# Expert weights loaded in DMAs of 128 columns

## What is computed

```python
xn = x / (np.linalg.norm(x, axis=-1, keepdims=True) + 1e-06)
logits = xn @ en.T / tau
expert_idx = np.argmax(logits, axis=1)
for e in range(E):
    mask = expert_idx == e
    h = np.maximum(x[mask] @ w1[e], 0.0)        # w1: 8 x 512 x 1024
    out[mask] = gate_w[mask, None] * (h @ w2[e]) # w2: 8 x 1024 x 512
```

## Time and profile before

| | us |
|---|---|
| median of 3 runs | 1424.7 |
| lowest and highest | 1419.62, 1425.99 |
| profiled execution, its own time | 1430.08 |
| profiled execution, span of the profile | 1428.4 |
| mean granted clock of PE (1 is 2.4 GHz) | 0.991 |

### The profile page before, as it was taken

One profiled execution on the slowest core, in us unless ns is written; L12 is line 12 of the kernel. 1 busy time (PEld: TensorE's weight loads), 2 busy tenths in 40 slices (PEclk: granted clock), 3 DMA queues, 4 the chain that ended last, 5 costly groups with the idle time before them and its releaser, 6 DMA issues.

```text
span 1428.4 us, 21354 instructions
## 1 busy us (share of the span) xinstructions
PE 1400.4 (98%) x7261; PEld 1151.3 (81%) x7261; DVE 805.0 (56%) x1498; ACT 686.0 (48%) x1016; POOL 699.8 (49%) x613
## 2 busy tenths in 40 slices
PE   8999999999999999999999999999999999998997
PEld 7888887887878878878888888888888788887886
DVE  7666786776757757767677486760002900075660
ACT  5333343443443533434435312545766666775664
POOL 5552243344353453443343332466666756586773
PEclk9999999999999999999999999899999999999999
DMA  8534243252352352432322122273434953369641
GB/s 254 167 117 144 54 104 85 58 129 72 74 117 61 83 130 61 105 86 51 84 60 45 67 74 67 89 235 83 97 83 113 236 149 90 77 150 240 141 115 27
DMA packets 200391, 152.54 MB, mean 107 GB/s; under 512 B 142812, under 2 KB 159196, under 8 KB 200160
## 3 DMA queue, kind: packets, MB, share of 16 engines
q1 hardware_dynamic: 59200, 99.20, 22.6%
q10 hardware_dynamic: 133056, 33.05, 14.1%
q0 software_dynamic: 8032, 18.93, 4.3%
HBM read 92.34 MB, written 29.43 MB: 85 GB/s over the span
## 4 chain that ended last, share of the span: by engine, by line
PE 81%; DMA 7%; POOL 4%; DVE 3%; issue 2%; ACT 2%; ACTq 0%; SPq 0%; DVEq 0%; POOLq 0%
PE y_ps L868 22%; PE h_ps L852 22%; PE y_ps L1009 15%; PE y_ps L975 15%; DMA shared<-in_v 3%; PE h_ps L812 2%; PE step_ps L768 2%; POOL g_lo L1858 2%; PE h_ps L987 2%; POOL shared L1839 1%; DVE weight_parts L1297 1%; DMA g_full<-shared 1%; DMA y_rows<-g_full 1%; DVE weight_parts L1292 1%; DMA shared<-shared 1%
## 5 line engine op out<-in xcount | busy, mean ns | idle before, releaser
L852 PE MATMUL h_ps<-x_hi_in,weight_parts 128*128 128x512 f32 x1144 | 373.5, 390 | 0.0
L868 PE MATMUL y_ps<-weight_parts,g_hi 128*128 128x512 f32 x1152 | 361.9, 395 | 7.8 <-POOL g_lo L1858 7.8
L1858 POOL TENSOR_TENSOR g_lo<-g_full,g_hi 128x512 fp32r<-128x512 f32 x144 | 202.7, 1408 | 322.1 <-ACT g_hi L1543 322.1
L868 PEld LDWEIGHTS y_ps<-weight_parts,g_hi 128*128 128x128 f32 x1152 | 213.2, 188 | 55.8 <-POOL g_lo L1858 10.8
L852 PEld LDWEIGHTS h_ps<-x_hi_in,weight_parts 128*128 128x128 f32 x1144 | 214.8, 188 | 44.4
L975 PE MATMUL y_ps<-weight_parts,x_hi_in 128*128 (+1 forms) x1032 | 244.5, 393 | 0.5 <-DVE weight_parts L1297 0.5
L1543 ACT ACTIVATE g_hi<-g_full 128x512 fp32r<-128x512 f32 x144 | 90.8, 631 | 294.5 <-PE y_ps L868 199.4
L975 PEld LDWEIGHTS y_ps<-weight_parts,x_hi_in 128*128 128x128 f32 x1032 | 194.9, 189 | 41.5 <-issue 1.2
L868 PE MATMUL y_ps<-weight_parts,g_lo 128*128 128x512 f32 x576 | 225.1, 391 | 0.0
L852 PE MATMUL h_ps<-x_lo_in,weight_parts 128*128 128x512 f32 x572 | 222.6, 389 | 0.0
L1164 DVE TENSOR_SCALAR g_full<-h_ps,alpha 128x512 f32<-128x512 f32 x144 | 107.9, 749 | 198.2 <-PE h_ps L852 197.6
(11 more groups left out here) (233 smaller groups left out, 1788.3 us busy)
## 6 DMA issues: line engine op xcount, KB each, us to landing
shared<-in_w SPq DMA_DIRECT2D x8, 2048.0 KB, 10.3
emb_all<-in_w SPq DMA_DIRECT2D x8, 2048.0 KB, 9.6
y_dram<-y_rows SPq DMA_DIRECT2D x9, 1024.0 KB, 4.4
shared<-in_q SPq DMA_DIRECT2D x34, 256.0 KB, 2.9
shared<-in_v SPq DMA_DIRECT2D x29, 288.0 KB
x_dram<-shared SPq DMA_DIRECT2D x32, 256.0 KB, 3.3
y_rows<-x_dram SPq DMA_DIRECT2D x32, 256.0 KB, 4.3
shared<-in_k SPq DMA_DIRECT2D x26, 288.0 KB, 3.8
```

What stands on the lines that cost most here:

```text
L852: mm = pe.matmul(h_ps[:, f % 2, :], w[:, k, f * P:(f + 1) * P], x[:, k, :], start=(n == 0), stop=(n == 3 * DC - 1))
L868: mm = pe.matmul(y_ps[:, j, :], a[:, f % 2, j * P:(j + 1) * P], w[:, f, :], start=(f == 0 and n == 0), stop=(f == FC - 1 and n == 2))
L1858: pool.tensor_tensor(gl[:, f % 2, :], g_full[:, f % 2, :], gh[:, f % 2, :].bitcast(F32), ALU.subtract).then_inc(gl_done, 1)
```

## The change

`load_expert` issues the 2 MB in blocks of 128 columns: eight DMAs of 256 KB for layer one, four DMAs of 512 KB for layer two. Every row of a block is 128 x 4 = 512 bytes, where the runs were 4 KB or 2 KB. Each block raises the same semaphore by 16, so that the waits for a load count 128 or 64 where they counted 16. The buffers, their layout, the order of loads and all other instructions are the same.

```diff
+RUN = 128
+BLOCKS = (EF // RUN, DM // RUN)
...
-                sp.dma_start((stage2 if layer else stage1).rearrange("p (c n) -> p c n", n=n),
-                             src[bass.ds(e, 1), :, :].rearrange("e (c p) n -> p (e c) n", p=P)).then_inc(e_w_loaded[layer], 16)
+                to = (stage2 if layer else stage1).rearrange("p (c n) -> p c n", n=n)
+                rows = src[bass.ds(e, 1), :, :].rearrange("e (c p) n -> p (e c) n", p=P)
+                for h in range(n // RUN):
+                    cols = slice(h * RUN, (h + 1) * RUN)
+                    sp.dma_start(to[:, :, cols], rows[:, :, cols]).then_inc(e_w_loaded[layer], 16)
...
-            dve.wait_ge(e_w_loaded[0], 16)
+            dve.wait_ge(e_w_loaded[0], 16 * BLOCKS[0])
...
-            dve.wait_ge(e_w_loaded[1], 16)
+            dve.wait_ge(e_w_loaded[1], 16 * BLOCKS[1])
...
-                dve.wait_ge(e_w_loaded[0], 16 * (r + 1))
+                dve.wait_ge(e_w_loaded[0], 16 * BLOCKS[0] * (r + 1))
...
-                dve.wait_ge(e_w_loaded[1], 16 * (r + 1))
+                dve.wait_ge(e_w_loaded[1], 16 * BLOCKS[1] * (r + 1))
...
-                act.wait_ge(e_w_loaded[layer], 16)
+                act.wait_ge(e_w_loaded[layer], 16 * BLOCKS[layer])
```

## The result

Beside the same runs of the kernel before (median 1426.18 us, 12 runs), the changed kernel took 1420.62 us (12 runs, 1415.06 to 1426.03). The ratio is 0.9964, with a 95% interval of 0.9946 to 0.9982: 5.1 us gained by the ratio, where 9.7 had been forecast, and less than the half per cent that the prediction named as its bound for "faster". The same kernel was timed three more times, each time beside the kernel before on the same chip: 0.9998, 0.9974 and 0.9993. Two of those four values lie outside the interval of the first, so the interval of one such timing understates the scatter. The mean of the four is 0.9982, some 2.5 us. That is the size that has to be explained.

What follows compares the result with a forecast made beforehand. TensorE (PE), 98% busy, was taken as the bound, with two stalls behind late transposes costing 4.13 + 6.63 = 10.76 us. Less 1 us for a remnant, 9.8 us off 1424.7 gives 1414.9, so 1415; range 1411 to 1431.

Steps and rivals of the forecast that it cites:

- The bound and its size: Expert stage: two PE stalls behind late column transposes, with lower clock after them, cost 10.76 us together.
- The price of the loads: Weight loads in 512-byte packets: 27 ns each, 6.9 us of every engine against 5.4, so 1.5 us more; issue hidden.
- the cover at the end: Last expert's final weight split ends 5.0 us before PE wants it, so loads 1.5 to 2.5 us later cost zero.
- The rival of slow loads: Short reads stream badly, 54 ns a packet; loads land after some 18 us; 1433 us, chance 0.20.
- The landing of a transpose: Late transposes in the expert stage land after 7.7 us, where they took 10.4 and 11.7.
- the pile-up of the earlier trace: From 1127.5 to 1133.5, after the load, two transposes, gathers and scatters needed 6 us, 53 ns a transpose packet.
- only partly: Rival: transposes, gathers and scatters still hold each other up; landings 8.5 to 10 us, 3 to 6 gained, 1420; chance 0.22.
- the tidy third case of the earlier trace: At 1309.9 to 1311.9 transpose and load packets alternate, 335 against 327; 18 ns a transpose packet, 85 a load packet.
- PE's tolerance: How late the two transposes may land before PE waits: 8.1 and 8.15 us after issue.
- both stalls just go: Likeliest case: both expert-stage stalls and their low clock vanish, 9.8 us gained after 1 us for a remnant; chance 0.36.
- The rest of the stage has PE back to back: Expert stage outside the two stalls: PE never waits, so 10.76 us is all the change can win.
- Order of arrival: Rival: later work waits for all of the load, both transposes land 1.5 us later; 1429; chance 0.22 including no effect.

Runs made afterwards that it cites:

- a1 to a3: The changed kernel unaltered, timed three more times against the kernel before: ratios 0.9998, 0.9974 and 0.9993.
- e2: The change's eight or four DMAs per load, but in runs of 2 KB; ratio to the kernel before 0.9978.
- e6: The change in layer-two loads alone, layer one still one DMA of 2 MB; ratio to the kernel before 0.9992.
- e13: 16 or 8 DMAs a load (128 and 256 KB) with runs of 1 or 2 KB; ratio to the kernel before 1.0010.
- e1: The kernel before, but experts 1 to 7 load only the first 128 rows of each matrix (wrong results); ratio to the kernel before 0.9921.
- e9: The change with blocks of 64 columns: 16 or 8 DMAs a load, runs of 256 bytes; ratio to the kernel before 0.9940.
- e12: Blocks of 64 columns run again: 16 or 8 DMAs a load, runs of 256 bytes; ratio to the kernel before 0.9963.
- e4: Each load in eight DMAs of 256 KB, runs of 2 KB, at most two outstanding; ratio to the kernel before 0.9968.
- e5: The change's blocks of 128 columns (512-byte runs), at most two outstanding; ratio to the kernel before 0.9976.
- e8: Eight DMAs of 256 KB, two outstanding, but the last expert's loads issued without waiting; ratio to the kernel before 0.9948.
- e10: The same kernel as e8 run again: two pieces of 256 KB outstanding, last expert free; ratio to the kernel before 0.9934.
- e11: As e8 but four pieces of 512 KB, two outstanding (1 MB), runs of 4 or 2 KB; ratio to the kernel before 0.9994.
- a1: The changed kernel unaltered, timed a second time against the kernel before; ratio 0.9998.

## Why the prediction was right in part, and wrong in its size

**The bound and its size: right.** Loads hold up the transposes, and this costs some 10 us. The version with small loads shows it, and the two later remedies win 5 to 8 us of it.

**The price of the loads: the packet right, the load too low.** A stretch of the changed kernel in which a load runs almost alone, 1281 to 1285 (DMA queues: packets, MB, share of 16 engines):

```profile
q1 hardware_dynamic: 2259, 1.14, 110.5%
q0 software_dynamic: 75, 0.02, 2.3%
```

1.105 x 4.0 x 16 / 2259 = 31 ns a packet; over all loads the median is 28 ns, the mean 32. 27 was forecast from the earlier trace rows. The page of the kernel before has this line for its packets:

```profile
DMA packets 200391, 152.54 MB, mean 107 GB/s; under 512 B 142812, under 2 KB 159196, under 8 KB 200160
```

So packets from 512 bytes to 2 KB rose from 159196 - 142812 = 16384 to 226013 - 144093 = 81920, by exactly the 65536 forecast. But from issue to last packet layer one took 9.8 us alone, where it was 7.3, so +2.5 and not +1.5, and beside other work 11.7 to 13.5 us. The load of layer two issued at 1137.87, behind one that was still running, took 15.6 us. That is over the 14 us which the prediction had named as a sign of being wrong. The term that was mis-sized is the issue. It had been put at 8 x 0.38 us, hidden. For the load that ran alone, SP's second DMA took 1.48 us to issue, and the engines were nearly empty from 826.4 to 827.4 (18.3% busy), which is 0.8 of the missing 1.0 us. SP's queue in the changed kernel:

```profile
1113.47 5.15 SPq L703 DMA_DIRECT2D emb_all<-in_w  x4
1126.56 6.87 SPq L703 DMA_DIRECT2D shared<-in_w  x8
1137.87 5.99 SPq L703 DMA_DIRECT2D emb_all<-in_w  x4
```

6.87 / 8 = 0.86 us and 5.99 / 4 = 1.5 us a DMA, where the earlier trace rows has 0.38: SP's queue is held up while it issues, by what the runs don't show. The single DMAs of layer one, duration in ns, least, median and most:

```profile
L703 SPq DMA_DIRECT2D shared<-in_w x64: 355/552/2492, 824.3 to 1337.9; - x64
```

For the time of the kernel this did no harm, as the cover at the end was kept. The last split of the changed kernel, and the first matmul that needs it:

```profile
1371.69 1.23 DVE L1302 TENSOR_TENSOR weight_parts<-emb_all,weight_parts 128x1024 fp32r<-128x1024 f32 x1
```

```profile
1377.88 0.62 PE L1014 MATMUL y_ps<-weight_parts,g_hi 128*128 x2
```

1377.88 - (1371.69 + 1.23) = 5.0 us, the very figure of before: that step holds. The rival of slow loads is refuted for the time of the kernel: the packet price is far from its 54 ns, and PE does not wait.

**The landing of a transpose: right in the mean, wrong where it counts.** The sum was 3.7 us to the first packet, 2.9 us of alternating, 1.1 us behind. The means over 34 transposes are 3.8 and 2.8. The 7.82 us at 1117.43 look like the forecast 7.7, but that is luck: its first packet came after 2.6 us, and 5.2 more went by to the landing, where 3.7 and 4.0 had been priced. And PE doesn't wait for the mean one. It waits for the worst, and the worst landed after 10.42 and 10.92 us. Here is the one issued at 1280.60: 4.6 us to its first packet and 6.3 from there to the landing. In the stretch just shown, 1281 to 1285, it has no packet at all, against 2259 of the load. Then, 1285.5 to 1290.5:

```profile
q10 hardware_dynamic: 1288, 0.32, 81.8%
q0 software_dynamic: 74, 0.17, 36.0%
q1 hardware_dynamic: 201, 0.09, 8.7%
```

0.818 x 5.0 x 16 / 1288 = 51 ns a transpose packet, and hardly any load left. This is the pile-up of the earlier trace rows over again (53 ns): transposes, gathers and scatters that all had to wait come together. The packets of the load being short does nothing for it. That was the rival "only partly", which gave 1420 us at a chance of 0.22, and its mechanism is what happened. Its size was 3 to 6 us, and the four timings give 2.5 in the mean; that the first median lay at 1420.62 was luck. The failed step is the price of the late transposes. I had measured the pile-up at 53 ns a packet in the earlier trace rows and then priced the alternation behind the first packet by the tidy third case of the earlier trace rows, 18 + 27 ns, so that both landed after 7.7 us, under PE's tolerance of 8.1, and "both stalls just go". The runs show the pile-up in its place, 51 ns a packet, landings of 10.42 and 10.92 us, and stalls of 2.50 and 2.11 us.

**"The rest of the stage has PE back to back": true of that execution only.** The second failed step is that no other transpose would become late. A stall also delays the next transposes, and so changes how they lie to the next loads. In the kernel before, the two transposes that followed the late one were issued at 1137.43 and 1150.17, 6.0 and 7.5 us behind the loads of 1131.48 and 1142.66, and landed in some 5 us. In the changed kernel the same two were issued at 1128.93 and 1140.88, 2.4 and 3.0 us behind the loads of 1126.56 and 1137.87, and landed after 8.28 and 10.42 us. So in these two profiles part of what is won at one transpose is given back at the next. It isn't shown that this holds from run to run: the kernel before, too, has four late pieces in its second profile, and the versions in between have 2 or 3 (a1 to a3, e2, e6, e13). What the versions without late pieces share is that their slowest transpose stays near PE's tolerance: 8.0 us in e1, 7.9 in e9 and e12, 7.7, 8.6, 7.9 and 7.3 in e4, e5, e8 and e10.

**Order of arrival.** This rival said that everything issued later waits for all of the load. For 4.0 us of the stretch above it looks like that even with packets of 512 bytes. The means say otherwise: a transpose begins 3.8 us after its issue in a load that lasts 12 us. What holds it for those 3.8 us the runs don't show. They show that it is no matter of the load's packet length alone (3.5 us at 2 and 4 KB, 3.8 at 512 bytes), and that it shrinks with what is outstanding: 2.9 us with 1 MB (e11) and 2.3 us with 512 KB (e4, e8 and e10). The Trainium skill ("DMA: Bandwidth & Descriptors", Queues, rings and completion order) says that each engine goes round the queues packet by packet, but its packet is a group of descriptors, 9 to 17 typically and at most 64, drained before the engine switches. The prediction took it for one of the profile's packets, and so had the rule let a transpose begin at once. If each of the profile's packets is one descriptor, which no run shows, the wait by that rule is an estimate of at most 64 x 85 ns = 5.4 us in the kernel before and 64 x 31 ns = 2.0 us in the changed one. The trace doesn't contradict the first (3.5 us in the mean, of which 1.2 are there without a load). The second is too short for the transpose of 1280.60, which waited 4.6 us.

**The profile's span.** The forecast took the saving off one execution's time and off the median alike. The span did fall by 7.6 us, but 5.56 us of this lay ahead of the expert stage. Read by span alone, the profile would have seemed to bear the forecast out.

The Trainium skill's rule of DMAs of 1 MiB or more ("DMA: Bandwidth & Descriptors", Rules for kernel authors) is given there for the highest bandwidth, and was named as speaking against the change. On bandwidth the trace agrees: layer one's load alone took 7.3 us as one DMA and 9.8 us as eight. For the time of this kernel it doesn't decide: eight of 256 KB, two at a time, gave the fastest version, since what limits this stage isn't how fast the loads run but what stands behind them. The prediction's 20.8 us for eight DMAs one after the other rests on a fit which that page has from DMAs issued by GpSimd, not SP. The changed kernel, whose eight overlap, stayed far below it.

## What to carry to other kernels

Where a bulk load and small urgent transfers share the DMA engines, limit what the load has outstanding (here 512 KB: some 8 us gained) rather than only its packet size (512 bytes: 2.5 us; 256 bytes, with twice the DMAs: 5 to 8 us), and leave it unlimited where the load itself is what is waited for. When a stall is to be removed, ask what the freed engine will meet next, since the stall may itself have kept later transfers apart from the next load. Count stalls over several profiles before summing them, and compare a stage by its own first and last instructions, not by the span.

## What the hardware showed that was not expected

- A DMA issued by ScalarE behind a 2 MB load of SP's queue has its first packet 3.5 to 3.8 us after its issue in the mean, and 1.2 to 1.3 us where it meets none; this didn't depend on whether the load's packets were 4 KB, 2 KB or 512 bytes.
- SP's issue of a DMA of 256 KB took 0.86 us in the mean of a load of eight, instead of 0.38 for a single DMA, and in the longest case 2.49 us.
- Packets of 256 bytes from DRAM cost 18 ns in the median (22 in the mean), of 512 bytes 28 (32). The halved blocks therefore need 512 x 22 = 11 us of each engine for a load where the change's need 256 x 32 = 8, and the kernel was still faster.
- The time that PE spent at its lower clock in the expert stage (its last microseconds left out) went from none (a1) to 20.4 us (the kernel before). The two profiles of the kernel before have 20.4 and 10.2 us of it, the four of the change 6.8 us, none, none and none. It lay behind stalls, which were in other places in every execution, and in nine of the 17 profiles also at the opening of the stage, between 905 and 929 us. So single executions of one kernel can differ by several us.
